# A chunk's first group of layer 1 slots moved between the second and the last third of its hidden product

## The reference

```python
# 1: linear attention with a sketched product feature map (4 batches, 4 heads, 1088 tokens, 32 channels)
q_p, k_p = (phi(q), phi(k))                       # phi: 8 x 8 products of two sketches
num, den = q_p @ (k_p.T @ v), q_p @ sum(k_p)
x = num / (den + 1e-06)
# 2: "layer 1": Fourier mixing over tokens and channels, norm, MLP 128 -> 512 -> 128
u = x + np.real(fft(fft(x, axis=1), axis=2))
un = (u - mu) / np.sqrt(var + 1e-06)
x2 = u + np.maximum(un @ w_ch1, 0.0) @ w_ch2
# 3: "layer 2": MLP 128 -> 1024 -> 128, gated by a convolution over tokens (3 taps per channel)
h = np.maximum(x2 @ w_in, 0.0)
conv_out = sum over k of conv_w[k] * (h moved by k - 1 tokens)
out = (h * 1.0 / (1.0 + np.exp(-conv_out))) @ w_out
```

## Time and profile before

| | us |
|---|---|
| median of three runs | 263.29 |
| the profiled execution | 263.48 |
| its span | 261.7 |
| TensorE busy | 249.6 (95%), 1524 matmuls |
| its weight loads | 211.2 (81%) |
| VectorE busy | 221.2 (85%) |
| ScalarE busy | 183.2 (70%) |
| GpSimd busy | 36.4 (14%) |

### The profile page before, as it was taken

One profiled execution on the slowest core, in us unless ns is written; L12 is line 12 of the kernel. 1 busy time (PEld: TensorE's weight loads), 2 busy tenths in 40 slices (PEclk: granted clock), 3 DMA queues, 4 the chain that ended last, 5 costly groups with the idle time before them and its releaser, 6 DMA issues.

```text
span 261.7 us, 4307 instructions
## 1 busy us (share of the span) xinstructions
PE 249.6 (95%) x1524; PEld 211.2 (81%) x1524; DVE 221.2 (85%) x391; ACT 183.2 (70%) x354; POOL 36.4 (14%) x90
## 2 busy tenths in 40 slices
PE   8999999999999999999959999998999999999985
PEld 6999999889899999988847777786778677777753
DVE  0747877997998789889999989989959999998992
ACT  2341435423576546577998998999989989978872
POOL 0000000000703333138980000000000000000000
PEclk9999999999999999999999999999999999999999
DMA  6958830210000000000000000002000002002002
GB/s 199 361 233 314 324 93 3 54 44 0 3 0 3 1 1 3 0 1 4 0 0 3 0 0 0 0 4 85 0 0 3 0 0 85 5 0 85 0 0 85
DMA packets 4341, 13.04 MB, mean 50 GB/s; under 512 B 736, under 2 KB 1504, under 8 KB 4320
## 3 DMA queue, kind: packets, MB, share of 16 engines
q1 hardware_dynamic: 4320, 12.77, 13.4%
HBM read 10.54 MB, written 2.23 MB: 49 GB/s over the span
## 4 chain that ended last, share of the span: by engine, by line
PE 78%; DVE 14%; ACT 5%; issue 3%; DVEq 0%; ACTq 0%
PE ps L590 20%; PE ps L511 9%; PE ps L513 8%; PE ps L512 8%; PE ps L428 6%; PE ps L504 5%; PE ps L440 5%; PE ps L551 4%; PE ps L469 4%; PE ps L453 3%; DVE arena L1018 3%; DVE arena L1023 2%; PE ps L596 2%; ACT arena L783 1%; DVE arena L933 1%
## 5 line engine op out<-in xcount | busy, mean ns | idle before, releaser
L590 PE MATMUL ps<-arena,wout 128*128 128x364 f32 (+1 forms) x192 | 62.9, 468 | 0.7 <-DVE arena L1030 0.7
L590 PEld LDWEIGHTS ps<-arena,wout 128*128 128x128 f32 x192 | 35.8, 189 | 20.8 <-issue 2.8
L783 ACT ACTIVATE arena<-ps 128x364 f32<-128x364 f32 x96 | 40.6, 479 | 5.0 <-PE ps L513 4.4
L1018 DVE SCALAR_TENSOR_TENSOR arena<-arena,taps 128x1088 f32<-128x1088 f32 x32 | 43.2, 1351 | 0.8 <-ACT arena L791 0.6
L1023 DVE SCALAR_TENSOR_TENSOR arena<-arena,taps 128x1088 f32<-128x1088 f32 x32 | 43.2, 1351 | 0.1
L1030 DVE TENSOR_TENSOR arena<-arena 128x1088 f32<-128x1088 f32 (+2 forms) x36 | 41.5, 1163 | 1.6 <-ACT arena L796 1.5
L511 PE MATMUL ps<-x2hi,wlo 128*128 128x364 f32 x96 | 39.6, 412 | 0.8 <-ACT arena L783 0.6
L796 ACT ACTIVATE arena<-arena 128x1088 f32<-128x1088 f32 x32 | 35.5, 1111 | 1.9 <-DVE arena L1023 1.9
L791 ACT ACTIVATE arena<-arena,taps 128x1088 f32<-128x1088 f32 x29 | 35.1, 1210 | 0.6
L513 PE MATMUL ps<-x2hi,whi 128*128 128x364 f32 x96 | 31.5, 328 | 0.0
L512 PE MATMUL ps<-x2lo,whi 128*128 128x364 f32 x96 | 31.5, 328 | 0.0
(11 more groups left out here) (82 smaller groups left out, 432.5 us busy)
## 6 DMA issues: line engine op xcount, KB each, us to landing
arena<-v_d SPq DMA_DIRECT2D x4, 594.0 KB, 3.9
arena<-qT_d SPq DMA_DIRECT2D x3, 545.0 KB, 6.9
arena<-kT_d SPq DMA_DIRECT2D x3, 544.5 KB, 6.0
out_d<-arena SPq DMA_DIRECT2D x3, 544.0 KB, 2.7
cos_t<-cos_d SPq DMA_DIRECT2D x1, 926.5 KB, 5.7
sin_t<-sin_d SPq DMA_DIRECT2D x1, 926.5 KB, 7.5
arena<-qT_d SPq DMA_DIRECT2D x2, 272.5 KB, 4.4
wraw<-w_d SPq DMA_DIRECT2D x2, 256.0 KB, 5.1
```

What stands on the lines that cost most here:

```text
L590: pe.matmul(ps[:, OUT_BANK + t, 0:z - a], wout[:, c, :], gate[:, i % GATES, a:z], start=(c == 0), stop=(c == C2 - 1)).then_inc(wout_done, 1)
L783: act.activation(h2[:, i % HIDDENS, t * TT:(t + 1) * TT], ps[:, bank_p(n), 0:TT], ACT.Relu).then_inc(h2_ready, 1)
L1018: dve.scalar_tensor_tensor(out=gate[:, i % GATES, 1:S + 1], in0=h2[:, i % HIDDENS, 0:S], scalar=taps[:, i % C2, 0:1], in1=gate[:, i % GATE ...
```

## The change

On TensorE the loop over the three thirds is opened up: the first two stand where all three stood, then the turns and the first group of slots, and then the last third. On ScalarE the turns and slots of the first group move from behind `relu(i)` to a place inside it, ahead of its third relu. The waits of each instruction are the same. A chunk without a slot or turn in its first group has the order that it had. VectorE's function isn't touched.

```diff
@@ TensorE, main loop
             for i in range(NI + FINAL_LAG):
                 if i < NI:
-                    for t in range(NT):
-                        hidden(i, t)
+                    hidden(i, 0)
+                    hidden(i, 1)
                 for r in turns_at(2 * i):
                     normed_transposes(r)
                 for n in slots_a(i):
                     slot(n)
+                if i < NI:
+                    hidden(i, 2)
                 for n in projects(i):
                     project(n)
@@ ScalarE, relu and main loop
             def relu(i):
                 for t in range(NT):
                     n = NT * i + t
+                    if t == 2:
+                        for r in turns_at(2 * i):
+                            normed_high(r)
+                        for m in slots_a(i):
+                            slot(m)
                     act.wait_ge(win_done, n + 1)
...
             relu(0)
-            for n in slots_a(0):
-                slot(n)
             for n in slots_b(0):
                 slot(n)
             for i in range(NI + 1):
                 if i + 1 < NI:
                     relu(i + 1)
-                    for r in turns_at(2 * i + 2):
-                        normed_high(r)
-                    for n in slots_a(i + 1):
-                        slot(n)
```

## The result

The changed kernel took 267.81 us (median of four runs, 267.5 to 268.3) against 263.12 us of the kernel before on the same chip: a ratio of 1.0179 with a 95% interval of 1.0163 to 1.0195, or 4.7 us. The forecast was 265.8 us with a range up to 267.3. The direction was right, the loss is almost twice what was forecast (2.46 us), and the time lies outside the range.

A forecast was written before the change was run, and what follows sets the result against it. VectorE was taken to bound chunks 0 to 5, TensorE the rest, with ScalarE close behind. Terms 1.04 + 0.50 + 0.64 - 0.22 + 0.50 = 2.46 us gave 265.8 us; range 263.5 to 267.3, its own 264.8 to 266.8.

The forecast's parts named there:

- steps 1, 2: Chunks 0 and 1: last thirds' relus come later, delaying VectorE's opening taps and so slot 27's "up", +1.04 us.
- (3): Chunk 5: one third now stands behind slot 27's wait for `unlo` instead of ahead of it, +0.50 us.
- (4): Chunk 8: its first third waits for the bank that ScalarE's late relu of chunk 7 empties, +0.64 us.
- (5): Chunk 8: slot 29's `x2hi` is written before the last relu, so slot 31's `unlo` is less late, -0.22 us.
- (6): Chunk 15: slot 34's earlier relu gains nothing lasting, and chunk 16's third now stands behind the `unlo` wait, +0.50 us.
- (7): Chunks 16 to 31: ScalarE's middle taps come up to 0.73 us later, but this isn't passed on, 0.
- step 1: Chunk 0: last third's end and relu come later, so VectorE's first opening tap is 0.95 to 1.0 us late.
- the clock: Rival, chance 0.05: TensorE's gap of some 3.3 us before slot 27 drops the clock, costing 2.3 us, 268.1 us total.
- The gaps close and nothing is late: Rival, chance 0.08: opening taps of chunks 0 and 1 aren't delayed and TensorE's later gaps shrink, giving 262.8 us.
- Only the first delay is passed on: Rival, chance 0.14: steps at chunks 5, 8 and 15 come to nothing as ScalarE catches up, giving 264.0 us.
- No change: Rival, chance 0.07: the 1.04 us delay is made up in TensorE's gaps behind chunk 6, giving 263.3 us.

The follow-up runs named there:

- E: Kernel before with the new order in all chunks but 0 and 1, plus 8 unread matmuls in the gap ahead of slot 27's "up": 265.07 us, ratio 1.0073.
- C: Changed kernel plus 12 unread matmuls in TensorE's gap ahead of slot 27's "up" in chunk 5: 266.20 us, ratio 1.0115 to the kernel before.
- A: Kernel before with the new order in chunks 0 and 1 alone: ratio 1.0083, six runs from 264.45 to 266.76 us.
- H: Kernel before with the new order in chunk 0 alone: one run, 266.43 us.
- J: Kernel before with the new order in chunk 1 alone: one run, 265.63 us.
- G: Kernel before with slot 27 moved from chunk 5 to behind chunk 6's three thirds, on TensorE and ScalarE: 262.18 us, ratio 0.9962.
- I: Kernel before with slot 27 moved behind chunk 6's thirds and the new order in chunks 8, 10, 12, 15 and 17 to 22: 262.28 us, ratio 0.9955.
- L: Kernel before with ScalarE's new order in all chunks and TensorE's old one: one run, 265.76 us.
- B: Kernel before with the new order in all chunks but 0 and 1: six runs, 265.17 to 269.23 us, median 267.94.
- D: Kernel before with the new order in chunk 5 alone: ratio 1.0121.
- K: Kernel before with TensorE's new order in all chunks and ScalarE's old one: one run, 269.96 us.
- F: Kernel before with the new order in the chunks from 8 on alone: 263.58 us, ratio 1.0008.

## Why the prediction was wrong, step by step

Lateness at chunk 31, from chunk 0 on, in us:

| | forecast | measured | from |
|---|---|---|---|
| slot 27's "up" late (steps 1, 2) | 1.04 | 1.61 | rows of after |
| chunk 5's third behind the wait (3) | 0.50 | 0.5 | E: 0.51 |
| the clock behind the gap | - | 1.41 | rows of after; C: 1.38 |
| chunk 8 waits for ScalarE (4) | 0.64 | 0.73 | chunks 6 to 8: 3.55, 4.28 |
| slot 29's `x2hi` earlier (5) | -0.22 | -0.28 | chunks 10 to 11 |
| chunks 15 to 17 (6) | 0.50 | 0.62 | 3.97 to 4.59 |
| chunks 17 to 31 (7) | 0 | 0.00 | 4.59 to 4.59 |
| sum | 2.46 | 4.59 | |

**Two things failed.** The first is step 1. It moved slot 23's "up" 0.50 us forward and took it that it could start there. I had looked up what waits for the moved instruction, not what the moved instruction itself waits for at its new place: bank 2, which group 6's `unhi` and `unlo` leave only 0.40 us later. The row that says so was in the trace of the kernel before (119.18), but not among my rows. It is worth 0.46 of the 0.57 us that the term was too small. Of the rest, 0.07 us stand in the chain above: from the end of the relu (121.73) to the tap (121.83) pass 0.10 us where I took 0.03. The last 0.04 stay open.

The second is that the clock was a rival with a chance of 0.05 and not a term of the sum; the runs show 1.4 us. The prediction had worked out the new gap and argued from a row that a gap of 1.73 us had passed at full clock. That row bounds the fall from one side only. That the gap came out as worked out (3.3 us; it was 3.17) is partly luck: the "up" was 0.57 us later than forecast, and TensorE itself reached chunk 5 0.66 us late, which the figure of 3.3 leaves out. The rival's own price, an estimate of 2.3 us for a stretch of 4.65, was too high. Its total of 268.1 us lies near the measured 267.8, also by luck, for two errors of opposite sign: 2.3 instead of 1.4, and 2.46 instead of 3.2 without the clock (C).

A slip without effect: an fp32 pair comes ahead of a moved third in 13 chunks and not 14, since chunk 0's "down" (slot 21) has three passes.

The Trainium skill's rule ("TensorE: Matmul & The Clock Gate", on HAM oscillation: a long idle gap throttles the clock again) is borne out in kind: 0.52 behind 3.17 us of idle time, 1.00 in the same program with the gap filled.

**The rivals.** "The gaps close and nothing is late" falls with the 1.49 us for which VectorE waits for the tap. "Only the first delay is passed on" falls with E, where 1.55 us stay although chunks 0 and 1 have the old order. "No change" falls with A, which has only the first delay: its chunk 7 is 3.24 us late and its chunk 31 still 3.05. In A, H and J the gaps behind chunk 7 take back 0.2 us and no more, between chunks 10 and 11; nothing of the delay is lost behind chunk 17 in any trace.

**Not tried:** a clock that is held without extra matmuls in the changed order, and the delay of chunk 0 with bank 2 free earlier. The 0.46 us of that wait are read from the rows of after, of A and of H (0.48 and 0.49 there), not from a run without it.

## What to carry to other kernels

An instruction that is moved forward has waits of its own; look up when each of its inputs is ready and when its output bank is free, not only who waits for it. Ahead of an engine's long wait, keep the work in front of the wait: a third moved behind it cost its own 0.5 us, and the longer gap cost the clock as well. If a program's bounding engine has one gap that is near the longest that its trace shows at full clock, then a change that makes it longer should be forecast with the clock's price as a term. Useless matmuls in the gap held the clock (C, E) but left both kernels slower than the one before; useful work moved into the gap (G and I) made the only gain.

## What the runs showed of the hardware

- The granted clock fell to the 1.2 GHz level at single gaps of TensorE of 3.17 us (changed kernel), 2.86 (H), 2.67 (L), 2.56 (B), 2.30 and 2.32 (A and J), 2.23 (D) and 2.18 (K). At 1.73 us in the kernel before and 1.70 in F the mean never lay more than 0.001 below full speed. Matmuls in the gap prevented it in all runs of C and E.
- The gap's length alone doesn't decide. In D the fall comes between 137.0 and 137.5 us, in a gap that began at 135.85: after at most 1.65 us of idle time, less than the 1.73 that passed. In A and H it comes as the "up" starts, in B some 1 us after it. What decides was not found.
- How much time is lost to it varies between runs of one kernel: B had means of 0.994, 0.987 and 0.980, and A fell in three of six runs. A step of the mean by 0.006 or 0.007 goes with some 2 us. By the traces one fall cost 1.4 us in the changed kernel and 1.6 in A, H and J.
- A fp32 matmul pair ahead of fp32r matmuls costs nothing that can be seen: six of the places that have it only in the new order are in chunks 17 to 22, and from there to chunk 31 the changed kernel stays 4.57 to 4.61 us late.
